# Attention with a score threshold and two gated feed-forward layers in fp32 on one core: another order of the first tile, scores in 64-column tiles, k in two halves, an early activation table, the last store in two pieces

## The reference, cut to what matters

```python
# q, k, v: (4, 8, 576, 64) fp32
scores = q @ k.T / 8                                   # per batch and head
thresh = scores.max(-1) - tau
attn = softmax(where(scores >= thresh, scores, -1e9))  # normalised with + 1e-9
x = (attn @ v)  ->  2304 tokens x 512
h = x @ w_in                                           # 512 -> 2048
y = (h * tanh(softplus(h))) @ w_out                    # mish, 2048 -> 512
g, val = y @ w_gate, y @ w_val                         # 512 -> 1536 each
out = (silu(g) * val) @ w_out2                         # 1536 -> 512
```

## Time and profile before

| | us |
|---|---|
| median of 3 runs | 1128.69 (1128.66 to 1129.42) |
| the profiled execution | 1129.18 |
| its span in the trace | 1127.3 |
| TensorE busy | 1108.6 (98%) |
| VectorE, ScalarE, GpSimd busy | 472.4, 459.3, 501.6 |

### The profile page before, as it was taken

How to read it: one execution, slowest core, us unless ns; L and a number is a source line. 1 busy time by engine, 2 the same in 40 slices (tenths; PEclk the granted TensorE clock), 3 DMA queues, 4 the chain that set the end, 5 groups by cost and what they waited for, 6 DMA issues and landing times.

```text
span 1127.3 us, 16940 instructions
## 1 busy us (share of the span) xinstructions
PE 1108.6 (98%) x6008; PEld 912.8 (81%) x6008; DVE 472.4 (42%) x939; ACT 459.3 (41%) x814; POOL 501.6 (44%) x688
## 2 busy tenths in 40 slices
PE   6999999999999999999999999999999999999998
PEld 3598888889888899887787778887787878888887
DVE  6636766521765762007554650036455510001210
ACT  6776555445544551344433440454343312401210
POOL 5677566645644663345334560454343322400220
PEclk9999999999999999999999999999999999999999
DMA  5487677888666788654454587554443456555552
GB/s 181 159 295 267 212 249 253 272 286 272 217 215 205 249 281 275 204 197 168 139 178 153 163 276 228 196 195 155 143 168 130 165 161 217 188 196 196 189 199 98
DMA packets 94626, 230.76 MB, mean 205 GB/s; under 512 B 16208, under 2 KB 31568, under 8 KB 94544
## 3 DMA queue, kind: packets, MB, share of 16 engines
q1 hardware_dynamic: 94400, 229.68, 61.6%
q10 hardware_dynamic: 144, 0.00, 0.0%
HBM read 189.27 MB, written 40.37 MB: 204 GB/s over the span
## 4 chain that ended last, share of the span: by engine, by line
PE 94%; DMA 3%; SPq 1%; DVE 1%; issue 1%; POOL 1%; ACT 1%; ACTq 0%; DVEq 0%
PE ps_m L729 24%; PE ps_m L731 24%; PE ps_m L730 24%; PE ps_x L802 6%; PE ps_x L828 5%; PE ps_s L757 3%; PE ps_s L771 2%; PE ps_s L772 2%; DMA w_raw<-weights 1%; PE ps_m L828 1%; DMA q_raw<-qt 1%; PE ps_x L824 1%; POOL p_t L1132 0%; PE ps_m L802 0%; DMA k_f<-kt 0%
## 5 line engine op out<-in xcount | busy, mean ns | idle before, releaser
L729 PE MATMUL ps_m<-x_hi,w_sp 128*128 128x512 f32 (+2 forms) x800 | 300.9, 376 | 2.8 <-ACT g_raw L949 1.7
L731 PE MATMUL ps_m<-x_hi,w_sp 128*128 128x512 f32 (+2 forms) x800 | 295.4, 369 | 0.0
L730 PE MATMUL ps_m<-x_lo,w_sp 128*128 128x512 f32 (+2 forms) x800 | 295.1, 369 | 0.0
L729 PE MATMUL ps_m<-g_hi,w_sp 128*128 128x512 f32 (+2 forms) x560 | 211.9, 378 | 0.1
L731 PE MATMUL ps_m<-g_hi,w_sp 128*128 128x512 f32 (+2 forms) x560 | 206.9, 369 | 0.0
L730 PE MATMUL ps_m<-g_lo,w_sp 128*128 128x512 f32 (+2 forms) x560 | 206.7, 369 | 0.0
L729 PEld LDWEIGHTS ps_m<-x_hi,w_sp 128*128 128x128 f32 x800 | 150.2, 188 | 32.0 <-issue 10.5
L1026 DVE SCALAR_TENSOR_TENSOR p_t<-ps_s,thr,p_t 128x576 f32<-128x576 f32 x144 | 116.4, 815 | 138.8 <-ACT p_t L926 127.4
L731 PEld LDWEIGHTS ps_m<-x_hi,w_sp 128*128 128x128 f32 x800 | 150.2, 188 | 22.2
L730 PEld LDWEIGHTS ps_m<-x_lo,w_sp 128*128 128x128 f32 x800 | 150.3, 188 | 19.5
L1019 DVE TENSOR_REDUCE nmax<-ps_s 128x1 f32<-128x576 f32 x144 | 107.3, 752 | 86.2 <-PE ps_s L772 72.3
(11 more groups left out here) (62 smaller groups left out, 1196.1 us busy)
## 6 DMA issues: line engine op xcount, KB each, us to landing
w_sp<-scratch SPq DMA_DIRECT2D x238, 512.0 KB, 3.3
scratch<-w_sp SPq DMA_DIRECT2D x68, 512.0 KB, 3.9
w_raw<-weights SPq DMA_DIRECT2D x102, 256.0 KB, 4.2
k_raw<-kt SPq DMA_DIRECT2D x56, 288.0 KB, 3.8
v_f<-v SPq DMA_DIRECT2D x64, 128.0 KB, 2.4
out_t<-o_sb SPq DMA_DIRECT2D x12, 256.0 KB, 4.0
k_f<-kt SPq DMA_DIRECT2D x8, 288.0 KB, 4.0
q_raw<-qt SPq DMA_DIRECT2D x8, 256.0 KB, 4.5
```

The costliest lines, as they stand in the source:

```text
L729: nc.tensor.matmul(ps, w_h, x_h, start=first, stop=False)
L730: nc.tensor.matmul(ps, w_h, x_l, start=False, stop=False)
L731: return nc.tensor.matmul(ps, w_l, x_h, start=False, stop=last)
```

## The change

- `FIRST_TILE`: other letter strings for all five queues. The letters are the same in number.
- `scores` in the first two tiles: every chunk is four matmuls of 64 queries by 288 keys, in tiles of 64x64.
- The host lays k down a second time with keys 0 to 287 on partitions 0 to 63 and keys 288 to 575 on partitions 64 to 127 (two versions, one for heads whose keys are rotated). The first two tiles load these 288 columns, 144 KB a head, where 576 columns, 288 KB, were loaded.
- A new step `warm` for each tile: a mish of one column with no wait, placed by the planner when the last `x_high` (first tile) or the last unit of the tile before is done. `exp` steps are held back from `warm` on.
- The planner's estimates: `scores` 0.56 for 0.6 and 0.7, `values` without its 10% and its 0.2, and 0.1 for each change between steps in 64-column tiles and others.
- The last output bank is copied in two pieces of 256 columns; SP's queue stores the left, ScalarE's queue the right one.

```diff
--- before.py
+++ after.py
@@ -140,6 +140,9 @@
+K_HALVES = slice(2 * SEQ - DH, 2 * SEQ - DH + HALF), slice(2 * SEQ - DH + HALF, 3 * SEQ - DH)
 def heads_in(C):
@@ -261,25 +264,31 @@
 SWITCH = 0.025
+SHAPE = 0.1
 PATIENCE = {"PE": 0.0, "ACT": 0.2, "DVE": 0.2, "POOL": 0.2, "SP": 0.0}
 
 FIRST_TILE = {
     "PE": ({"s": "scores", "t": "tpose", "v": "values"},
-           "sssssstttsstttsstvtvtstsvvtvststtttsvsvvtttstsvttvtstsvvvtvtttvttttvvvvv"),
+           "sssssstttsstttssvvtttssvtttvsstttvstsvtttvvssvvtttstsvvvtttvttvttttvvvvv"),
     "ACT": ({"q": "q_scaled", "e": "exp", "c": "p_copy", "h": "x_high", "w": "w_high"},
-           "qqeewwqeewqweeqccceeccqceeccqceechccececcqceecccceechcceeccccchcccwwcwh"),
+           "qqeewwweeqqweecccweecccqeecqcceeqccceechccceeqccceechccceeccccchcccwcwh"),
     "DVE": ({"r": "rowmax", "m": "mask", "i": "recip", "l": "x_low"},
-           "rrmmirirmmirirmmririmmirirmmrirmimirlrmimriirmmirirmmilrirmmiill"),
+           "rrmmirrimmirrmmiririmmirirmmirrimmirrimmilrrimmirrimmilrirmmiill"),
     "POOL": ({"t": "thresh", "e": "eps", "n": "norm", "w": "w_low"},
-           "tteettnenenttweentntenentntwewtetnewntetnenetntneenttneentnteennwww"),
+           "ttewetntnentetwenetntenentntewetntnewtetnenenttneenttnewentnteennww"),
     "SP": ({"q": "load_qk", "v": "load_v", "w": "load"},
-           "qqqqwwwvvvwqqqvwvqwvwvv"),
+           "qqqqwvvwwwqwqvvqwqvwvvv"),
 }
 
 def matmul_time(n):
     return max(0.112, 0.008 + n / 2300)
+def tiled(k):
+    return k[0] == "values" or k[0] == "scores" and 2 * CHUNK[k[1]][0] < WHOLE_HEADS
@@ -309,7 +318,7 @@
                 add("SP", 0.8, 2, ("load_qk", H), (("scores", last_chunk(before)) if before >= 0 else None, 0.1))
-                add("ACT", 0.2 + 0.00096 * n, 5, ("q_scaled", H), (("load_qk", H), 2.6))
+                add("ACT", 0.2 + 0.00096 * n, 5, ("q_scaled", H), (("load_qk", H), 3.6 if H == 0 else 2.6))
                 add("SP", 0.8, 2, ("load_v", H), (v_used, 0.1))
@@ -333,7 +342,7 @@
                     ends += [(("q_scaled", H), near), (("q_low", H), near), (("k_low", H), near)]
-                time = (0.6 if alone else 0.7) if whole else 0.53 * len(heads_in(C))
+                time = 0.56 if whole else 0.53 * len(heads_in(C))
                 add("PE", time, 0 if alone else 1, ("scores", C), (("mask", C - 2), near), (pace, 0.0), *ends)
@@ -354,13 +363,13 @@
                     ends = [(("p_copy", J, i), near) for i, (_, keys) in enumerate(turns) if key in keys]
-                    add("PE", 1.1 * (n / 600 + 0.02), 0, ("values", J, key), (("load_v", 2 * J + 1), 3.0),
+                    add("PE", n / 600 + 0.02, 0, ("values", J, key), (("load_v", 2 * J + 1), 3.0),
                         (("x_low", 0, j - 1), near), *ends)
                 add("ACT", 0.17 + 0.00084 * n, 2, ("x_high", 0, j), (("values", J, KC - 1), 0.3))
                 add("DVE", 0.17 + 0.00101 * n, 3, ("x_low", 0, j), (("x_high", 0, j), 0.2))
                 continue
             ends = [(("p_copy", J, i), near) for i in range(len(turns))]
-            add("PE", 0.2 + KC * (n / 600 + 0.05), 0, ("values", J, 0), (("load_v", 2 * J + 1), 3.0),
+            add("PE", KC * (n / 600 + 0.05), 0, ("values", J, 0), (("load_v", 2 * J + 1), 3.0),
                 (self.x_free(USE0[J] + len(turns)), near), *ends)
@@ -398,6 +407,7 @@
         act, dve, pool = 0.17 + 0.00084 * N, 0.17 + 0.00101 * N, 0.1 + 0.00236 * N
+        add("ACT", 0.22, 0, ("warm", m), (("x_high", 0, DC - 1) if m == 0 else unit_end(UNITS * m - 1), 0.0), table="mish")
         for u in range(UNITS):
@@ -472,8 +482,8 @@
         turn = dict.fromkeys(names, 0)
-        table, mished = "exp", 0
-        out, last_pe = [], None
+        table, mished, in_mish = "exp", 0, False
+        out, last_pe, in_tiles = [], None, False
         fixed = {e: [kinds[letter] for letter in letters] for e, (kinds, letters) in FIRST_TILE.items()}
@@ -482,7 +492,7 @@
                     kind = self.step[k][5]
-                    if kind == "exp" and mished % FC1:
+                    if kind == "exp" and in_mish:
                         continue
@@ -496,10 +506,11 @@
             mished += k[0] == "mish"
+            in_mish = k[0] == "warm" or in_mish and not (k[0] == "mish" and mished % FC1 == 0)
             free[e] = t + self.step[k][1]
             if e == "PE":
-                free[e] += SWITCH * ((k[0] == "tpose") != (last_pe == "tpose"))
-                last_pe = k[0]
+                free[e] += SWITCH * ((k[0] == "tpose") != (last_pe == "tpose")) + SHAPE * (tiled(k) != in_tiles)
+                last_pe, in_tiles = k[0], tiled(k)
             out.append((t, len(out), k))
@@ -554,8 +566,8 @@
         g_raw, _ = sb("g_raw", [P, FC1, BANK], F32, over=spot)
-        k_f, _ = sb("k_f", [P, SLOTS, SEQ], F32, over=spot)
-        q_f, _ = sb("q_f", [P, SLOTS, TILES[0]], F32, over=spot + 4 * SLOTS * SEQ)
+        k_f, _ = sb("k_f", [P, SLOTS, HALF], F32, over=spot)
+        q_f, _ = sb("q_f", [P, SLOTS, TILES[0]], F32, over=spot + 4 * SLOTS * HALF)
         w_raw, _ = sb("w_raw", [P, W_RAW, UW * P])
@@ -601,7 +613,7 @@
-            return (q_f[:, H % SLOTS], k_f[:, H % SLOTS]) if H < ALONE_HEADS else (q_raw[:, H % 2], k_raw[:, H % 2])
+            return (q_f[:, H % SLOTS], k_f[:, H % SLOTS]) if H < ALONE_HEADS else (q_raw[:, H % 2], k_raw[:, H % 2, 0:HALF])
@@ -648,6 +661,14 @@
         block = ctx.enter_context(nc.Block())
+        def left_of(m, d):
+            return TILES[m] // 2 if (m, d) == (len(TILES) - 1, DC - 1) else TILES[m]
+        def k_halves(head, H):
+            return kt[head, :, K_HALVES[keys_of(H).start > 0]]
@@ -659,14 +680,17 @@
                     sp.dma_start(q_f[:, slot, :], qt[head, :, q0:q0 + n]).then_inc(q_f_loaded[slot], 16)
-                    sp.dma_start(k_f[:, slot, :], kt[head, :, keys_of(H)]).then_inc(k_f_loaded[slot], 16)
+                    sp.dma_start(k_f[:, slot, :], k_halves(head, H)).then_inc(k_f_loaded[slot], 16)
                     return
                 slot = H % 2
                 if split(H) >= 2:
                     sp.wait_ge(k_ready, split(H) - 1)
                 elif woven(H) >= 2:
                     sp.wait_ge(s_filled, last_chunk(H - 2) + 1)
-                sp.dma_start(k_raw[:, slot, :], kt[head, :, keys_of(H)]).then_inc(k_loaded[slot], 16)
+                if H < WHOLE_HEADS:
+                    sp.dma_start(k_raw[:, slot, 0:HALF], k_halves(head, H)).then_inc(k_loaded[slot], 16)
+                else:
+                    sp.dma_start(k_raw[:, slot, :], kt[head, :, keys_of(H)]).then_inc(k_loaded[slot], 16)
                 if split(H) >= 2:
@@ -704,8 +728,9 @@
                 sp.wait_ge(out_ready, DC * m + d + 1)
-                cols = slice(sum(TILES[:m]), sum(TILES[:m + 1]))
-                sp.dma_start(out_t[d, :, cols], o_sb[:, d % 2, 0:TILES[m]]).then_inc(stored[d % 2], 16)
+                width = left_of(m, d)
+                cols = slice(sum(TILES[:m]), sum(TILES[:m]) + width)
+                sp.dma_start(out_t[d, :, cols], o_sb[:, d % 2, 0:width]).then_inc(stored[d % 2], 16)
@@ -750,12 +776,11 @@
                         rows = slice(half * DH, (half + 1) * DH)
-                        for H in heads_in(C):
-                            q, k = qk_of(H)
-                            left = n * (H % 2)
-                            q0, q1 = max(b * P, left), min((b + 1) * P, left + n)
-                            last = nc.tensor.matmul(s_banks(C)[q0 - b * P:q1 - b * P, half, :], q[rows, q0 - left:q1 - left],
-                                                    k[rows, half * HALF:(half + 1) * HALF], start=True, stop=True)
+                        for to in (slice(0, DH), slice(DH, P)):
+                            odd, at = divmod(b * P + to.start, n)
+                            q, k = qk_of(2 * J + odd)
+                            last = nc.tensor.matmul(s_banks(C)[to, half, :], q[rows, at:at + DH],
+                                                    k[rows], start=True, stop=True)
                 else:
@@ -944,6 +969,9 @@
+            def warm():
+                act.activation(warmed, q_scale, ACT.Mish)
             def mish(m, f):
@@ -972,6 +1000,13 @@
                 act.activation(w_sp[:, slot, 0, :], w_raw[:, r % W_RAW, :], ACT.Copy).then_inc(w_hi_ready, 1)
+            def keep_right():
+                m, d = len(TILES) - 1, DC - 1
+                right = slice(left_of(m, d), TILES[m])
+                act.wait_ge(right_ready, 1)
+                cols = slice(sum(TILES[:m]) + right.start, sum(TILES))
+                act.dma_start(out_t[d, :, cols], o_sb[:, d % 2, right]).then_inc(right_stored, 16)
@@ -1003,6 +1040,7 @@
                     w_high(*args)
+            keep_right()
@@ -1073,7 +1111,10 @@
                     dve.wait_ge(stored[d % 2], 16 * ((DC * m + d) // 2))
-                dve.tensor_copy(o_sb[:, d % 2, 0:TILES[m]], m_bank(m, N_O + d)).then_inc(out_ready, 1)
+                width = left_of(m, d)
```

(13 more changed lines are left out.)

## The result

The changed kernel takes 1120.61 us, the median of four executions (1120.13 to 1121.0); the kernel before 1128.70 in the same comparison. The ratio is 0.9927, 95% interval 0.9909 to 0.9944: 8.1 us less, where 4.4 had been forecast (1124.3, range 1122.0 to 1127.4). Repeated on two other chips the ratio was 0.9932 both times, 7.7 us less.

A forecast was written before the change was run, and what follows sets the result against it. TensorE, busy 98% of the span, was taken as the bound. First tile 1.9, second tile's scores 0.7, mish 1.5 and end 0.3 make 4.4 us off 1129.18: 1124.8, or 1124.3 for the median; range 1122.0 to 1127.4.

The forecast's parts named there:

- The early table: At the second tile's first mish: loading ScalarE's table earlier removes TensorE's 1.7 us wait; 1.5 us taken.
- 64x64 tiles: Scores of the first two tiles: each chunk takes 0.65 us for 0.69; 0.3 us less in the first, 0.7 in the second.
- Rival (d): Scores in the first two tiles: 64x64 weight loads stand in a row, 12 us, giving 1137.3; chance 0.03.
- Rival (c): At three changes of tile: held-back exps end attention late, 2.3 us each, 7.0 in all, giving 1131.3; chance 0.06.
- The order of the first tile: First tile on TensorE: nine fewer changes of step kind save 1.5 us, less 0.3 for chunks that may be late.
- rival (e): At the start: the third weight lands late and all is 2.4 us later, giving 1126.7; chance 0.10.
- The norms: First tile, GpSimd's string: norm 2 ends earlier, so the first transpose no longer waits for it; 0.4 us less.
- First tile in sum: First tile: reordering 1.5, less 0.3 for late chunks, plus 0.4 for norms and 0.3 for 64x64 scores: 1.9 us less.
- k in halves behind the start, and the planner's estimates: After the first k, TensorE waits for no k, so halves cost nothing; new estimates reorder woven steps, given no gain.
- Rival (a): Woven stages: the new order brings waits as large as the known ones, 3.2 us, giving 1127.5; chance 0.13.
- The end: Last output copy and store in two pieces: 0.3 us less, bounds 0.5 less and 0.15 more.
- Rival (b): First tile: VectorE, not TensorE, sets the pace, so fewer entries give nothing and the tile brings 0.4: 1125.8; chance 0.12.

The follow-up runs named there:

- the mended start: Changed kernel with the third weight split moved behind the exps of chunks 2 and 3: ratio 0.9929; with GpSimd's second weight split also moved later: 0.9930.

## Why the prediction was wrong, step by step

The direction was right and so were the mechanisms of the four terms; the sum was half of what came, and the time lay outside the range. The step that failed is the price of two terms. The early table was priced at the wait that the list shows (1.5), and took 2.6 us off alone. The 64x64 tiles were given nothing ahead of chunk 8, and 0.7 of the first tile's 1.0 was there. And the start was compared with the wrong time.

- **64x64 tiles, forecast 1.0.** Measured alone 2.1 (0.8 to 3.5), left out 1.3. In the second tile 0.83 against 0.7. In the first 1.0 against 0.3: I had given the gain only to the ten chunks at the full rate, where it was 0.32, and no term to the stretch ahead of it. How much of the 0.7 there is the edit's and how much the execution's stays open. The sentence that the clock reads 1.00 there was wrong in itself: there was no record to read. Rival (d) is refuted.
- **The early table, forecast 1.5.** This is the largest error in the sum. Measured 2.6 alone and 2.1 left out, and its place in the order is enough. The wait of 1.7 was read rightly and went, but I priced it as idle time alone. Behind it stand 0.7 us of longer pitch (in four of five traces) and 0.4 of scores, and in one of five the clock at half rate. Rival (c), held-back exps, did not happen: in eleven traces with the early table the longest wait behind the first unit was 1.84 us.
- **The order of the first tile, forecast 1.5 less 0.3.** In its own stretch 1.15 and 1.26, as forecast. What failed is the step at the start. By bytes I had put exp 2 between 11.5 and 12.0; it was 12.06, and 11.95 and 11.90 in the repeats, so that was read rightly. But I set it against the 11.78 of before and called the start even, while the chain had moved 0.7 ahead: with the old strings exp 2 runs at 10.77. I had looked at the third weight alone, and the second is issued behind v as well. k gave 0.7 and the strings took 1.2 (0.9 to 1.2 in the third pair's start over the traces): rival (e), in half its size and together with the forecast instead of in its place.
- **The norms, forecast 0.4.** The transposes follow chunk 5 in after without a wait, and the 0.39 is gone. But in after without the strings the start is sooner with a wait of 0.49. It isn't the norms that set the start. The wait for norm 4, which was to stay, went from 0.50 to 0.68.
- **First tile in sum, forecast 1.9.** 2.2 in the first pair of traces; 2.2 to 3.2 over the five traces with after's first tile (52.75 to 53.50) against 55.7 and 56.0.
- **k in halves behind the start, and the planner's estimates, forecast nothing.** Right within what can be told (0.9994; 0.9931 for 0.9932). Rival (a) was the wrong side of this: waits behind the first unit other than the mish's were 2.5 and 2.0 us in the two traces of before and 1.5, 2.6 and 2.0 in the three of after. They move with every execution and did not grow. In the first pair of traces they fell by 1.0 us, which no term had forecast; it is luck.
- **The end, forecast 0.3.** 0.24.
- **Rival (b).** Refuted: fewer entries did shorten the stretch, TensorE was what was late.

The single terms measured alone make 2.1 + 2.6 + 0.7 + 0.2 = 5.6 us, and after without strings and estimates, which is these four together, 6.4 (0.9943). Against the 7.7 of the repeats that leaves 1.2 for the reordering, with intervals that overlap; in before the same reordering took 3.8 off, most of it at the mish, so the terms don't add up as independent ones. The first result, 8.1, was 0.4 above its repeats. The range failed because each of its ends came from one wait or one chunk in one trace: no end below 1122.0 was open to "the wait costs more than it shows". (By its own terms the forecast's lower end is 1122.7 and not 1122.6.)

Open: what sets the pitch of 202.5 or 206.7 ns. It is not one edit alone: not the order (after, unchanged, had both), nor the k halves, nor the 32 bytes by which the new tile shifts SBUF (before with the early table had 206.7 in the last stretch). And whether the mended start would be worth 1 us over many executions.

## What to carry to other kernels

A wait of the bounding engine can cost more than its own length: count the rate at which that engine resumes, from the starts of its next instructions, and bound it upward. In a hand-written order, an instruction that waits for a DMA must not stand ahead of one on the chain: nine saved changes of kind (1.2 us) were paid for at the start (0.9 to 1.2 us), by a weight issued behind v and a split too many ahead of an exp. And take two traces of the kernel before: of its four waits one was 1.5 us in the first and 0.4 in the second. Last, a clock of 1.00 means something only where the trace has a record of the clock.

## What the runs showed of the hardware

- In stretches with nothing between, matmuls of 448 columns follow one another at 202.5 or at 206.7 ns, and hold that over up to some 15 units; 512-column ones at 226.7 in all seventeen traces.
- A wait of 2.10 us was followed by 3.4 us at a granted clock of 0.50; waits of 1.6 to 1.8 us at the same place were not.
- In the first 16 to 22 us a pair of score chunks takes 2.20 us for 1.13 later, and transposes start 213 ns apart for 109. The trace has no clock record there (the column reads 1.00), and its first record stands where the rate rises, between 16.85 and 22.03 us in sixteen traces.
- Four fp32 matmuls of 64x64 by 288 columns take 0.65 us standing alone, two of 64x128 0.69.
- The switch of ScalarE's table took 1.28 us and nothing on either side: the activation before ends 0.02 us ahead of it, and where the next one is ready it starts 0.01 us behind. The Trainium skill, ScalarE: Activation LUTs, section What ACT_TABLE_LOAD costs, states 1283 ns for the load, which the trace agrees with, and about 1380 ns more for a drain, which no trace here shows.
